# First expert's weights fetched in the last coupled step, the wait at the seam moved to GpSimd, and the weight remainders of the start spread anew

## The chip, the cores and the metric

One core of one Trainium2 chip runs the whole kernel in one launch. The metric is the device time of that launch in microseconds (us), and less is better. The kernel before was run three times: 968.25, 970.22 and 970.82 us, so its median is 970.22.

## The reference

Three layers, one after the other, all in fp32:

```python
# 1: decayed linear attention, 4 batches x 8 heads x 768 steps x 48 channels
for t in range(S):
    S_re, S_im = ar * S_re - ai * S_im + k[t] (x) v[t],  ar * S_im + ai * S_re
    y[t] = q[t] @ S_re                  # a normalised to at most 0.999 in size
# 2: dense MLP on 3072 tokens, 384 -> 2048 -> 384
h = x @ w_in;  g = max(h, 0) + alpha * min(h, 0);  x2 = g @ w_out
# 3: routed MLP: tokens with x2 @ w_skip > 0 go to one of 8 experts (384 -> 1024 -> 384)
e = argmax(x2 @ w_gate)
out = x2 + prob[e] * (relu(x2 @ w1[e]) @ w2[e])     # others: out = x2
```

## The kernel before, in words

The kernel has two blocks of instructions, one after the other; a barrier of all engines stands at the end of each. The border between them is called the seam here.

**Phase 1** (`phase1`) does the attention and the dense MLP, on 8 "halves" of 384 tokens, each of 3 chunks of 128. Step h does the attention of half h, the MLP of half h-1 and the preparation of the gates of half h+1. The order of the work of each engine is written out by hand in a function `step` of each engine. Step 0 has no MLP, steps 1 to 6 are a loop of three turns, step 7 is the last coupled step (there is no half 8 to prepare), and then the MLP of half 7 runs alone. All transfers of phase 1 are issued by SyncE, in order: q, k and v of a chunk (`load_qkv`), the decayed q and k into the layout of TensorE (`move_qk`, 10 transfers), the attention's result (`move_y`, 6), the state (`move_state`, 4), and the rows of x2, into `out` and into the scratch tensor `x2_rows` (`store_x2`, L378 and L379).

**The start of phase 1** fills the MLP's weights. Every weight is kept as two fp32r parts, a high part that ScalarE rounds and a remainder that VectorE subtracts. There are 22 pieces in a fixed order, `WEIGHT_ORDER`: in0, in1, out0, out1, in2, out2, out3, in3, out4, out5, in4, out6, out7, in5, and then out8 to out15. A piece of w_in has 512 KB and one of two staging buffers, a piece of w_out comes as two transfers of 192 KB and has one of three. So the chain of an out piece is: SyncE issues its transfers as soon as the remainder of the piece three before it is taken (`load_pack`), TensorE makes its gate columns, ScalarE makes the side-scaled copy and the high part (`split_pack`, L742 to L746), VectorE the remainder (`low_weights`, L1027). Between the pieces VectorE prepares the gates of half 0: three `scale_gates` (a reciprocal and two products, one for each chunk), seven `within`, four `across`, three `carry_products`, then `sum_products` of ScalarE's squares, `inverse` (a reciprocal, L870) and `decay_qk` (L879, L885) for the first chunk. In the kernel before VectorE takes one remainder behind each of those steps, and three, three and two behind the three `carry_products`; ScalarE makes all 22 high parts, then the three squares (L627), then `take_factors` (L623).

**The seam.** SyncE issues the last two stores of x2 and then waits for both to land; only after that does it reach the barrier that all the other engines have been waiting at.

**Phase 2** (`phase2`) routes. VectorE finds the place of each token, TensorE builds with 48 matmuls (L1274) a table of the tokens of each "slot" of 128 tokens of one expert; GpSimd gathers the rows of slot 1 by an indirect transfer into `x_in` (L1595); TensorE turns them (L1280), multiplies by w1 (L1303) and by w2 (L1317); GpSimd gathers slot s+1 while slot s is computed, and scatters finished slots (L1599). Each expert's w2 is split into high part (ScalarE, L1349) and remainder (VectorE, L1514) as well. The weights of an expert, 1.5 MB of w1 (L1248) and 1.5 MB of w2 (L1251), are issued by SyncE into one of four pairs of buffers: experts 0 to 2 at the start of phase 2, expert 3 when the table is full, because parts of the table's inputs (`in_row`, `entries`) lie in its buffers; experts 4 to 7 as experts finish. There are 13 slots in this data; the first two belong to expert 0.

```python
            for p in range(BODY - 1):
                load(0, p)
            sp.wait_ge(table_full, 1)
            load(0, BODY - 1)
```

Of the kernel before, what the change touches and what calls it, by code (L numbers as in the profile page):

```python
# [12 lines left out]
P = 128  # L13
# [99 lines left out]
def build(nc, qk, v, a, mask_in, w_in, w_pack, alpha, w_skip, w_gate, w1, w2, out, x2_rows):  # L113
    with ExitStack() as ctx:
        def sem(name):
            return ctx.enter_context(nc.semaphore(name))

        def sb(name, shape, dt=F32):
            return ctx.enter_context(nc.sbuf_tensor(name, shape, dt))

        mlp_ps = [ctx.enter_context(nc.psum_tensor(f"mlp_ps{i}", [P, 512], F32)) for i in range(2)]
        out_ps = [ctx.enter_context(nc.psum_tensor(f"out_ps{i}", [P, 512], F32)) for i in range(3)]
        att_ps = [ctx.enter_context(nc.psum_tensor(f"att_ps{i}", [P, 512], F32)) for i in range(3)]

        ident = sb("ident", [P, P])
        logits = sb("logits", [P, NT, LANES])

        phase1(nc, qk, v, a, mask_in, w_in, w_pack, alpha, w_skip, w_gate, out, x2_rows,
               mlp_ps, out_ps, att_ps, ident, logits)
        phase2(nc, w1, w2, out, x2_rows, mlp_ps, out_ps, att_ps, ident, logits)  # L130


def phase1(nc, qk, v, a, mask_in, w_in, w_pack, alpha, w_skip, w_gate, out, x2_rows,
           mlp_ps, out_ps, att_ps, ident, logits):
    with ExitStack() as ctx:
        def sem(name):
            return ctx.enter_context(nc.semaphore(name))

        def sb(name, shape, dt=F32):
            return ctx.enter_context(nc.sbuf_tensor(name, shape, dt))  # L140
# [10 lines left out]

        gates = [sb(f"gates{i}", [P, 2, NC * DM]) for i in range(2)]
        sq = sb("sq", [P, 2, NC * DM])
# [4 lines left out]

        qk_raw = sb("qk_raw", [P, 2, KT, 2, CH])
        qk_dec = sb("qk_dec", [P, 2, KT, 2, CH])  # L160
# [14 lines left out]
        g_parts = sb("g_parts", [P, 4, 2, HT], F32R)  # L175
        x2 = sb("x2", [P, NC, DL])

# [68 lines left out]
        x2_taken = sem("x2_taken")  # L246
        x2_stored = sem("x2_stored")


# [45 lines left out]
        def _(sp):  # L295
# [20 lines left out]
            def load_qkv(h, c):  # L316
# [13 lines left out]
                sp.dma_start(qk_raw[:, m, :, :, :].rearrange("p t w s -> p (t w s)"), q_src).then_inc(qk_loaded[m], 16)  # L330
                sp.dma_start(v_nat[:, m, :], v_src).then_inc(v_loaded[m], 16)
# [98 lines left out]
            with sp.Fori(0, 3) as i:  # L430
# [7 lines left out]
                step(Half(i, 2), True, True, load_but_last)  # L438
            step(Half(0, HALVES - 1), True, False, lambda: None)
            store_x2(Half(0, HALVES - 1))  # L440
            sp.wait_ge(x2_stored, val(32 * HALVES + 1))

# [151 lines left out]
        def _(act):  # L594
# [164 lines left out]
            for c in range(NC):  # L759
                pad_gates(Half(0, 0), c)  # L760
            for kind, n in WEIGHT_ORDER:
                if kind == "in":
                    split_w_in(n)
                else:
                    split_pack(n)
            for c in range(NC):
                square_products(Half(0, 0), c)
            take_factors(Half(0, 0))
            act.wait_ge(wo_lo, NF)
# [12 lines left out]
        def _(dve):  # L782
# [89 lines left out]
            def decay_qk(h, c):  # L872

                g_ = chunk_no(h, c)
                m, loads = buffer_of(h, c)
                dve.wait_ge(qk_loaded[m], loads)
                dve.wait_ge(f_inverted, val(g_ + 1))
                k_ = qk_raw[:, m, :, 1, :]
                dve.tensor_tensor(k_, k_, tiles(of_chunk(inv[:, :], c)), ALU.mult).then_inc(k_scaled, 1)  # L879
                if back(h, c):  # L880
                    dve.wait_ge(qk_moved, val(g_ * (32 * len(OP_MOVES))))
                dve.wait_ge(k_scaled, val(g_ + 1))
                for r in range(2):
                    G = tiles(of_chunk(gates[h.p][:, r, :], c)).unsqueeze(2).broadcast_to([P, KT, 2, CH])
                    last = dve.tensor_tensor(qk_dec[:, r, :, :, :], qk_raw[:, m, :, :, :], G, ALU.mult)  # L885
                last.then_inc(qk_made, 1)
# [169 lines left out]
            dve.tensor_tensor(slope_side[:, :], slope[:, :], side[:, :], ALU.mult).then_inc(alpha_made, 1)  # L1056
            scale_gates(first_h, 0)
            low_weights(0, 1)
            scale_gates(first_h, 1)
            low_weights(1, 2)  # L1060
            scale_gates(first_h, 2)
            low_weights(2, 3)
            for j in range(1, SL):
                within(first_h, j)
                low_weights(2 + j, 3 + j)
            for k in range(len(STEP_SHIFTS)):
                across(first_h, k)
                low_weights(10 + k, 11 + k)
            for part in range(3):
                carry_products(first_h, part)  # L1070
                low_weights(14 + 3 * part, 17 + 3 * part)
            for c in range(NC):
                sum_products(first_h, c)
            inverse(first_h, 0)
            decay_qk(first_h, 0)
            inverse(first_h, 1)
            inverse(first_h, 2)
# [30 lines left out]

def phase2(nc, w1, w2, out, x2_rows, mlp_ps, out_ps, att_ps, ident, logits):
    with ExitStack() as ctx:  # L1110
# [6 lines left out]

        w1_v = [sb(f"w1_sb{p}", [P, KT, FE]) for p in range(BODY)]
        w2_raw = [sb(f"w2_raw{p}", [P, NFE, DM]) for p in range(BODY)]
        w2_v = [[sb(f"w2_{part}{p}", [P, NFE, DM], F32R) for part in ("hi", "lo")] for p in range(BODY)]  # L1120
# [47 lines left out]
        scatter_at = sb("scatter_at", [P, 1], I32)  # L1168
        x_in = sb("x_in", [P, DM])
        x_kept_rows = sb("x_kept_rows", [P, 2, DM])  # L1170
        xT = sb("xT_e", [P, KT, P])
        hT = sb("hT", [P, 2, NFE, P], F32R)
        y = sb("y", [P, DM])

# [16 lines left out]
        pads_made = sem("pads_made")  # L1191
        w1_loaded = [sem(f"w1_loaded{p}") for p in range(BODY)]
        w2_loaded = [sem(f"w2_loaded{p}") for p in range(BODY)]
        w2_hi = sem("w2_hi")
# [47 lines left out]
        def _(sp):  # L1242
# [10 lines left out]

            for p in range(BODY - 1):
                load(0, p)
            sp.wait_ge(table_full, 1)
            load(0, BODY - 1)
# [318 lines left out]
        def _(pool):  # L1576
# [123 lines left out]
```

## Time and profile before

| what | value |
|---|---|
| three runs | 968.25, 970.22, 970.82 us |
| the profiled execution: its own time | 968.83 us |
| its span, first to last instruction | 966.9 us |
| what lies outside the span | 1.9 us |
| mean granted TensorE clock | 0.922 of 2.4 GHz |
| TensorE matmul, VectorE, ScalarE, GpSimd busy | 751.7, 699.2, 367.4, 51.8 us |
| phase 1, to the barrier at the seam | 0 to 766.4 us |
| routing, up to the first slot's first matmul | 766.4 to 805.1 us |
| the 13 slots | 805.1 to 966.9 us |

All times in the rows are counted from the start of the span. A line number is that of the kernel before. "SPq" is the queue of transfers that SyncE issues; the time beside such an entry is that of issuing, not that of the transfer. In the chain of waits each piece is followed back from the last instruction to what released it.

### The profile page before, as it was taken

How to read it: one execution, taken by the hardware profiler on the slowest of the kernel's cores; microseconds unless marked ns; L12 is line 12 of the kernel's file. 1: busy time of each engine (PE TensorE's matmuls, PEld its weight loads, DVE VectorE, ACT ScalarE, POOL GpSimd, SP SyncE). 2: the span in 40 equal slices, each digit the busy share in tenths (PEclk: the TensorE clock that was granted, in tenths of full speed). 3: DMA queues.
4: the chain of work that ended last, by engine and by line, in shares of the span. 5: the costliest groups of instructions: out<-in, count | busy, mean ns of one | idle time of the engine just before them, and what ended most of it. 6: DMA issues, size and time to landing. Idle time of an engine off the chain costs nothing. (4 is left out here: it accounts for less than half of the span.)

```text
span 966.9 us, 16131 instructions
## 1 busy us (share of the span) xinstructions
PE 751.7 (78%) x5478; PEld 723.3 (75%) x5479; DVE 699.2 (72%) x1231; ACT 367.4 (38%) x805; POOL 51.8 (5%) x48
## 2 busy tenths in 40 slices
PE   1343456987897989889798889979999547998786
PEld 1333456987886989788688788879999447998786
DVE  6967988988999799898899989875333373434333
ACT  5452234435434534433453353334433222322221
POOL 1000000000000000000000000000000012233122
PEclk9999567999999899999999999999999857999799
DMA  6542343243342424424242352233210393324520
GB/s 188 178 152 79 93 118 90 64 130 113 80 109 62 139 65 115 126 66 133 70 118 73 100 151 63 70 113 97 57 56 1 133 357 110 126 73 163 205 82 17
DMA packets 82433, 104.74 MB, mean 108 GB/s; under 512 B 15990, under 2 KB 68384, under 8 KB 82336
## 3 DMA queue, kind: packets, MB, share of 16 engines
q1 hardware_dynamic: 80544, 99.69, 35.2%
q0 software_dynamic: 1792, 3.76, 1.2%
q8 instruction: 61, 1.00, 0.4%
q14 instruction: 36, 0.29, 0.1%
HBM read 61.04 MB, written 12.19 MB: 76 GB/s over the span
## 5 line engine op out<-in xcount | busy, mean ns | idle before, releaser
L524 PE MATMUL out_ps<-w_out_hi,g_parts 128*128 128x394 f32 x768 | 225.3, 350 | 26.3 <-DVE g_parts L933 26.3
L514 PE MATMUL mlp_ps<-xT,w_in_hi 128*128 128x384 f32 x768 | 207.1, 351 | 20.3 <-DMA xT<-y_parts 8.6
L524 PEld LDWEIGHTS out_ps<-w_out_hi,g_parts 128*128 128x128 f32 x768 | 145.9, 193 | 30.3 <-DVE g_parts L933 30.2
L514 PEld LDWEIGHTS mlp_ps<-xT,w_in_hi 128*128 128x128 f32 x768 | 140.5, 194 | 27.5 <-issue 13.5
L928 DVE SCALAR_TENSOR_TENSOR g<-mlp_ps,slope_side,bent 128x384 f32<-128x384 f32 x128 | 78.6, 615 | 83.4 <-ACT bent L666 75.3
L524 PE MATMUL out_ps<-w_out_lo,g_parts 128*128 128x394 f32 x384 | 133.8, 348 | 0.0
L514 PE MATMUL mlp_ps<-xT,w_in_lo 128*128 128x384 f32 x384 | 131.2, 342 | 0.0
L666 ACT ACTIVATE bent<-mlp_ps,bend_size 128x384 f32<-128x384 f32 x128 | 73.7, 576 | 149.5 <-PE mlp_ps L514 149.0
L1303 PE MATMUL mlp_ps<-xT_e,w_sb 128*128 128x128 f32 x624 | 79.5, 290 | 19.3 <-issue 14.1
L1303 PEld LDWEIGHTS mlp_ps<-xT_e,w_sb 128*128 128x128 f32 x624 | 77.4, 205 | 22.1 <-issue 16.9
L672 ACT ACTIVATE g_parts<-g 128x384 fp32r<-128x384 f32 x128 | 66.2, 517 | 35.4 <-DVE g L928 35.4
L468 PE MATMUL att_ps<-ident,kq 112*128 112x112 f32 x192 | 27.5, 295 | 60.8 <-DMA kq<-qk_dec 60.8
L1544 DVE SCALAR_TENSOR_TENSOR hT<-mlp_ps,hT 128x256 fp32r<-128x256 f32 x52 | 21.8, 424 | 72.8 <-ACT hT L1375 72.8
L524 PEld LDWEIGHTS out_ps<-w_out_lo,g_parts 128*128 128x128 f32 x384 | 74.1, 193 | 0.0
L514 PEld LDWEIGHTS mlp_ps<-xT,w_in_lo 128*128 128x128 f32 x384 | 74.1, 193 | 0.0
L660 ACT ACTIVATE s_t<-s_in,f_pair 112x96 f32<-112x96 f32 x192 | 53.6, 362 | 52.9 <-DVE s_in L912 34.1
L468 PEld LDWEIGHTS att_ps<-ident,kq 112*128 112x128 f32 x192 | 22.9, 160 | 65.5 <-DMA kq<-qk_dec 55.2
L933 DVE TENSOR_TENSOR g_parts<-g,g_parts 128x384 fp32r<-128x384 f32 x128 | 70.3, 549 | 0.3
L459 PE MATMUL att_ps<-kq 112*128 112x128 f32 x384 | 60.5, 320 | 5.3 <-ACT k_back L634 5.3
L798 DVE RECIPROCAL sq<-sq 128x384 f32<-128x384 f32 x24 | 61.1, 2547 | 1.2 <-ACT sq L614 1.2
L459 PEld LDWEIGHTS att_ps<-kq 112*128 112x128 f32 x384 | 57.1, 234 | 6.4 <-ACT k_back L634 6.4
L870 DVE RECIPROCAL inv<-norms 128x384 f32<-128x384 f32 x24 | 60.0, 2529 | 0.0
(150 smaller groups left out, 1082.8 us busy)
## 6 DMA issues: line engine op xcount, KB each, us to landing
kq<-qk_dec SPq DMA_DIRECT2D x96, 144.0 KB, 3.0
w_sb<-in_w SPq DMA_DIRECT2D x8, 1536.0 KB, 7.7
w_raw<-in_w SPq DMA_DIRECT2D x8, 1536.0 KB, 12.0
gates<-in_a SPq DMA_DIRECT2D x24, 384.0 KB, 4.3
qk_raw<-in_qk SPq DMA_DIRECT2D x24, 384.0 KB, 4.2
xT<-y_parts SPq DMA_DIRECT2D x48, 144.0 KB, 2.8
v_nat<-in_v SPq DMA_DIRECT2D x24, 192.0 KB, 4.0
out<-x SPq DMA_DIRECT2D x8, 576.0 KB, 3.2
```

The lines of the kernel that those rows point to most:

```text
L459: last = pe.matmul(ps[:, n * CH:(n + 1) * CH], kq[:, slot, 1, :], kq[:, slot, 0, :], start=True, stop=True)
L468: last = pe.transpose(ps[:, n * ROWS:(n + 1) * ROWS], kq[:, PAIRS * half + n, 1, :], ident[0:ROWS, 0:ROWS])
L514: last = pe.matmul(ps[:, 0:HT], w_in_v[s][:, kk, f * P:(f + 1) * P], xT[n.p][:, kk, m, :], start=(kk == 0 and j == 0), stop=(kk == KT - 1 ...
L524: last = pe.matmul(out_ps[i][:, 0:DL], g_parts[:, f % 4, s, i * P:(i + 1) * P], w_out_v[m][:, f, :], start=(f == 0 and j == 0), stop=(f == ...
L660: last = act.activation(s_t[:, r, :, pair_, :], s_in[:, :, pair_, :], ACT.Copy, scale=f_pair[:, h.p, pair_, c, r:r + 1])
L666: act.activation(bent[:, f % 2, :], mlp_ps[f % 2][:, 0:HT], ACT.Relu, scale=bend_size[:, f:f + 1]).then_inc(bent_made, 1)
L672: act.activation(g_parts[:, f % 4, 0, :], g[:, f % 3, :], ACT.Copy).then_inc(g_hi, 1)
L798: dve.reciprocal(s1, s0).then_inc(norm_inv, 1)
L870: dve.reciprocal(of_chunk(inv[:, :], c), of_chunk(norms[:, :], c)).then_inc(f_inverted, 1)
L928: dve.scalar_tensor_tensor(out=g[:, f % 3, :], in0=mlp_ps[f % 2][:, 0:HT], scalar=slope_side[:, f:f + 1], in1=bent[:, f % 2, :], op0=ALU.m ...
L933: dve.tensor_tensor(g_parts[:, f % 4, 1, :], g[:, f % 3, :], g_parts[:, f % 4, 0, :].bitcast(F32), ALU.subtract).then_inc(g_lo, 1)
L1303: last = pe.matmul(mlp_ps[g % 2][:, (f % 2) * P:(f % 2 + 1) * P], w1_v[p][:, kk, f * P:(f + 1) * P], xT[:, kk, :], start=(kk == 0), stop=( ...
```

## The change

- The buffers of expert 0 (`arena`, two of 12 KB for each partition) are allocated outside both phases. In phase 1 they hold `gates` and `qk_raw`, both buffers of each, so that phase 2 needs no memory of its own for them; `x2` shares `rows` with `x_in`, `x_kept_rows` and `y`.
- SyncE issues the 3 MB of expert 0 in step 7, after `move_state` of chunk 1, behind a wait for the last `decay_qk`.
- SyncE no longer waits for the last stores. GpSimd waits for them in phase 2, ahead of the first gather.
- Phase 2 starts with the loads of experts 1 and 2. Expert 3 is issued when the first gather has landed instead of when the table is full.
- The clearing of `y` on GpSimd stands behind the first gather.
- In the start of phase 1 VectorE takes two remainders behind each `scale_gates` and one behind each later step; one (out14) stands between the first and the second `sum_products`, and the last (out15) behind `decay_qk` of chunk 0. ScalarE makes 20 high parts, the three squares, the last two high parts, and then `take_factors`.

```diff
+        arena = [sb(f"arena{i}", [P, KT * FE]) for i in range(2)]
+        rows = sb("rows", [P, NC * DL + DM])
+        x2_stored = sem("x2_stored")
+        first_loaded = [sem(f"first_loaded{i}") for i in range(2)]
...
-        gates = [sb(f"gates{i}", [P, 2, NC * DM]) for i in range(2)]
+        gates = [arena[i][:, 0:2 * NC * DM].rearrange("p (r x) -> p r x", r=2) for i in range(2)]
...
-        qk_raw = sb("qk_raw", [P, 2, KT, 2, CH])
+        qk_raw = [arena[i][:, 2 * NC * DM:2 * NC * DM + 2 * KT * CH].rearrange("p (t w s) -> p t w s", t=KT, w=2)
+                  for i in range(2)]
...
-        x2 = sb("x2", [P, NC, DL])
+        x2 = rows[:, 0:NC * DL].rearrange("p (i d) -> p i d", i=NC)
...
-            step(Half(0, HALVES - 1), True, False, lambda: None)
+            def fetch_first_expert():
+                sp.wait_ge(qk_made, NC * HALVES)
+                sp.dma_start(arena[0][:, :].rearrange("p (k f) -> p k f", k=KT),
+                             w1[0:1].rearrange("e (k p) f -> p (e k) f", p=P)).then_inc(first_loaded[0], 16)
+                sp.dma_start(arena[1][:, :].rearrange("p (f d) -> p f d", f=NFE),
+                             w2[0:1].rearrange("e (f p) d -> p (e f) d", p=P)).then_inc(first_loaded[1], 16)
+
+            step(Half(0, HALVES - 1), True, False, fetch_first_expert)
             store_x2(Half(0, HALVES - 1))
-            sp.wait_ge(x2_stored, val(32 * HALVES + 1))
...
-            for kind, n in WEIGHT_ORDER:
-                if kind == "in":
-                    split_w_in(n)
-                else:
-                    split_pack(n)
+            split_weights(0, 20)
             for c in range(NC):
                 square_products(Half(0, 0), c)
+            split_weights(20, 22)
             take_factors(Half(0, 0))
...
-            scale_gates(first_h, 0)
-            low_weights(0, 1)
-            scale_gates(first_h, 1)
-            low_weights(1, 2)
-            scale_gates(first_h, 2)
-            low_weights(2, 3)
+            for c in range(NC):
+                scale_gates(first_h, c)
+                low_weights(2 * c, 2 * c + 2)
             for j in range(1, SL):
                 within(first_h, j)
-                low_weights(2 + j, 3 + j)
+                low_weights(5 + j, 6 + j)
             for k in range(len(STEP_SHIFTS)):
                 across(first_h, k)
-                low_weights(10 + k, 11 + k)
+                low_weights(13 + k, 14 + k)
             for part in range(3):
                 carry_products(first_h, part)
-                low_weights(14 + 3 * part, 17 + 3 * part)
-            for c in range(NC):
-                sum_products(first_h, c)
+                low_weights(17 + part, 18 + part)
+            sum_products(first_h, 0)
+            low_weights(20, 21)
+            sum_products(first_h, 1)
+            sum_products(first_h, 2)
             inverse(first_h, 0)
             decay_qk(first_h, 0)
+            low_weights(21, 22)
...
-            for p in range(BODY - 1):
+            for p in range(1, BODY - 1):
                 load(0, p)
-            sp.wait_ge(table_full, 1)
+            sp.wait_ge(x_gathered, 16)
             load(0, BODY - 1)
...
-            pool.memset(y[:, :], 0.0).then_inc(pads_made, 1)
+            pool.wait_ge(x2_stored, 32 * HALVES + 1)
...
-            pool.wait_ge(pads_made, 2)
+            pool.wait_ge(pads_made, 1)
             pool.wait_ge(first_at, 2)
             gather()
+            pool.memset(y[:, :], 0.0).then_inc(pads_made, 1)
```

## Rows read from the trace of the kernel before

**Rows 1.** The page, transfer issues: w2's loads, count, KB each, us to landing.
```profile
w_raw<-in_w SPq DMA_DIRECT2D x8, 1536.0 KB, 12.0
```

**Rows 2.** The chain of waits from the table to slot 2: start us, us, what.
```profile
782.35 10.52 PE att_ps L1274 x48
...
794.48 8.75 DMA x_in<-x_rows,gather_at
...
805.06 7.30 PE mlp_ps L1303 x48
...
816.93 5.36 PE mlp_ps L1303 x48
```

**Rows 3.** The timeline of SyncE's queue over the seam: start us, us of issuing, line.
```profile
762.06 0.49 SPq L379 DMA_DIRECT2D x_rows<-x  x1
766.68 0.38 SPq L1248 DMA_DIRECT2D w_sb<-in_w  x1
```

**Rows 4.** SyncE's waits, 640 to 967 us: us in total, times, longest.
```profile
SPq L135 <- DMA x_rows<-x: 3.7, 1, 3.7
```

**Rows 5.** 2 us of gather 1: busy of five engines, TensorE's clock, DMA share, GB/s.
```profile
798.00:800.00 2.00, 0.00 (x0) 0.00 (x0) 0.00 (x0) 0.00 (x0) 0.00 (x0) 0.50 1.04 394
```

**Rows 6.** GpSimd's timeline: gathers 1, 2 and 8.
```profile
794.48 3.27 POOL L1595 DMA_INDIRECT x_in<-x_rows,gather_at  x1 [25.14 <-issue]
805.13 1.00 POOL L1595 DMA_INDIRECT x_in<-x_rows,gather_at  x1 [7.38 <-PE att_ps L1280]
...
868.47 1.02 POOL L1595 DMA_INDIRECT x_in<-x_rows,gather_at  x1 [4.42 <-DVE x_kept_rows L1510]
```

**Rows 7.** Issue to landing of gathers 1, 3, 5, 8 (issued 794.48, 814.62, 834.74, 868.47).
```profile
x_in<-x_rows,gather_at POOLq DMA_INDIRECT x1, 8.8
...
x_in<-x_rows,gather_at POOLq DMA_INDIRECT x1, 5.2
...
x_in<-x_rows,gather_at POOLq DMA_INDIRECT x1, 9.2
...
x_in<-x_rows,gather_at POOLq DMA_INDIRECT x1, 6.2
```

**Rows 8.** The waits of 0 to 100 us: us in total, times, longest.
```profile
PE att_ps L468 <- DMA kq<-qk_dec: 24.6, 2, 16.8
...
DVE w_out_lo L1027 <- ACT w_out_hi L746: 6.8, 6, 1.7
```

**Rows 9.** VectorE's timeline: remainders of out0 and out1, then the end of the start.
```profile
26.53 0.56 DVE L1027 TENSOR_TENSOR w_out_lo<-x,w_out_hi 128x394 fp32r<-128x394 f32 x1
...
28.42 0.57 DVE L1027 TENSOR_TENSOR w_out_lo<-x,w_out_hi 128x394 fp32r<-128x394 f32 x1
...
62.93 1.14 DVE L858 TENSOR_TENSOR gates<-norms,inv 128x945 f32<-128x945 f32 x1
...
66.72 0.57 DVE L1027 TENSOR_TENSOR w_out_lo<-x,w_out_hi 128x394 fp32r<-128x394 f32 x1 [1.00 <-ACT w_out_hi L746]
...
69.39 2.54 DVE L870 RECIPROCAL inv<-norms 128x384 f32<-128x384 f32 x1
...
72.63 1.83 DVE L885 TENSOR_TENSOR qk_dec<-qk_raw,gates 128x768 f32<-128x768 f32 x2
```

**Rows 10.** ScalarE's timeline: high part of out3, then the squares.
```profile
31.57 0.18 ACT L742 ACTIVATE x<-mlp_ps 128x10 f32<-128x10 f32 x1 [6.89 <-PE mlp_ps L569]
...
32.43 0.53 ACT L746 ACTIVATE w_out_hi<-x 128x394 fp32r<-128x394 f32 x1
...
66.59 2.29 ACT L627 ACTIVATE sq<-gates 128x768 f32<-128x768 f32 x3
```

**Rows 11.** SyncE's queue in step 7, around the place of the fetch.
```profile
683.67 2.97 SPq L367 DMA_DIRECT2D s_stack<-state  x4
695.42 4.60 SPq L359 DMA_DIRECT2D xT<-y_parts  x6
```

**Rows 12.** TensorE's timeline at the loop's way back, between experts 3 and 4.
```profile
898.45 8.35 PE L1303 MATMUL mlp_ps<-xT_e,w_sb 128*128 128x128 f32 x48 [6.80 <-issue]
```

More of the change, by code:

```diff
@@ L126, in build, with phase1 @@
         logits = sb("logits", [P, NT, LANES])
[L128 to L134, printed above, removed]
+        arena = [sb(f"arena{i}", [P, KT * FE]) for i in range(2)]
+        rows = sb("rows", [P, NC * DL + DM])
+        x2_stored = sem("x2_stored")
+        first_loaded = [sem(f"first_loaded{i}") for i in range(2)]
+        phase1(nc, qk, v, a, mask_in, w_in, w_pack, alpha, w_skip, w_gate, w1, w2, out, x2_rows,
+               mlp_ps, out_ps, att_ps, ident, logits, arena, rows, x2_stored, first_loaded)
+        phase2(nc, w1, w2, out, x2_rows, mlp_ps, out_ps, att_ps, ident, logits, arena, rows, x2_stored, first_loaded)
+def phase1(nc, qk, v, a, mask_in, w_in, w_pack, alpha, w_skip, w_gate, w1, w2, out, x2_rows,
+           mlp_ps, out_ps, att_ps, ident, logits, arena, rows, x2_stored, first_loaded):
     with ExitStack() as ctx:
@@ L246, in phase1 @@
         x2_taken = sem("x2_taken")
-        x2_stored = sem("x2_stored")
         def att(h, name, c):
@@ L329, in load_qkv @@
                     v_src = v[bass.ds(n, 1), :, :].rearrange("n p x -> (n p) x")
-                sp.dma_start(qk_raw[:, m, :, :, :].rearrange("p t w s -> p (t w s)"), q_src).then_inc(qk_loaded[m], 16)
+                sp.dma_start(qk_raw[m].rearrange("p t w s -> p (t w s)"), q_src).then_inc(qk_loaded[m], 16)
                 sp.dma_start(v_nat[:, m, :], v_src).then_inc(v_loaded[m], 16)
@@ L760, in _, with split_weights @@
                 pad_gates(Half(0, 0), c)
-            for kind, n in WEIGHT_ORDER:
-                if kind == "in":
-                    split_w_in(n)
-                else:
-                    split_pack(n)
+            def split_weights(first, last):
+                for kind, n in WEIGHT_ORDER[first:last]:
+                    if kind == "in":
+                        split_w_in(n)
+                    else:
+                        split_pack(n)
+            split_weights(0, 20)
             for c in range(NC):
                 square_products(Half(0, 0), c)
+            split_weights(20, 22)
             take_factors(Half(0, 0))
@@ L877, in decay_qk @@
                 dve.wait_ge(f_inverted, val(g_ + 1))
-                k_ = qk_raw[:, m, :, 1, :]
+                k_ = qk_raw[m][:, :, 1, :]
                 dve.tensor_tensor(k_, k_, tiles(of_chunk(inv[:, :], c)), ALU.mult).then_inc(k_scaled, 1)
@@ L884, in decay_qk @@
                     G = tiles(of_chunk(gates[h.p][:, r, :], c)).unsqueeze(2).broadcast_to([P, KT, 2, CH])
-                    last = dve.tensor_tensor(qk_dec[:, r, :, :, :], qk_raw[:, m, :, :, :], G, ALU.mult)
+                    last = dve.tensor_tensor(qk_dec[:, r, :, :, :], qk_raw[m][:, :, :, :], G, ALU.mult)
                 last.then_inc(qk_made, 1)
@@ L1106, in _, with phase2 @@
                                pattern=[[-1, P]], channel_multiplier=1).then_inc(consts, 1)
-def phase2(nc, w1, w2, out, x2_rows, mlp_ps, out_ps, att_ps, ident, logits):
+def phase2(nc, w1, w2, out, x2_rows, mlp_ps, out_ps, att_ps, ident, logits, arena, rows, x2_stored, first_loaded):
     with ExitStack() as ctx:
@@ L1115, in sb @@
             return ctx.enter_context(nc.sbuf_tensor(name, shape, dt))
-        w1_v = [sb(f"w1_sb{p}", [P, KT, FE]) for p in range(BODY)]
-        w2_raw = [sb(f"w2_raw{p}", [P, NFE, DM]) for p in range(BODY)]
+        w1_v = [arena[0][:, :].rearrange("p (k f) -> p k f", k=KT),
+                *(sb(f"w1_sb{p}", [P, KT, FE]) for p in range(1, BODY))]
+        w2_raw = [arena[1][:, :].rearrange("p (f d) -> p f d", f=NFE),
+                  *(sb(f"w2_raw{p}", [P, NFE, DM]) for p in range(1, BODY))]
         w2_v = [[sb(f"w2_{part}{p}", [P, NFE, DM], F32R) for part in ("hi", "lo")] for p in range(BODY)]
@@ L1168, in phase2 @@
         scatter_at = sb("scatter_at", [P, 1], I32)
-        x_in = sb("x_in", [P, DM])
-        x_kept_rows = sb("x_kept_rows", [P, 2, DM])
+        x_in = rows[:, NC * DL:NC * DL + DM]
+        x_kept_rows = rows[:, 0:2 * DM].rearrange("p (a d) -> p a d", a=2)
         xT = sb("xT_e", [P, KT, P])
         hT = sb("hT", [P, 2, NFE, P], F32R)
-        y = sb("y", [P, DM])
+        y = rows[:, 2 * DM:3 * DM]
         step = sem("step")
@@ L1191, in phase2 @@
         pads_made = sem("pads_made")
-        w1_loaded = [sem(f"w1_loaded{p}") for p in range(BODY)]
-        w2_loaded = [sem(f"w2_loaded{p}") for p in range(BODY)]
+        w1_loaded = [first_loaded[0], *(sem(f"w1_loaded{p}") for p in range(1, BODY))]
+        w2_loaded = [first_loaded[1], *(sem(f"w2_loaded{p}") for p in range(1, BODY))]
         w2_hi = sem("w2_hi")
```

## The prediction

> **What bounds the kernel now.** I read the chain of waits first, since it names what ends last at each point, then the timelines of the queues at the three places that the change touches, then the waits. The chain is one string over the whole span: nothing in the kernel waits for a fixed point in time, so a microsecond taken out of the string at one place is a microsecond off the end, as long as nothing that was hidden comes up beside it. Three links of the string are touched.
>
> *The start.* TensorE has nothing to do in step 0 until the decayed q and k arrive: it waits 16.8 us for them in one piece [rows 8]. Ahead of those transfers stands VectorE: last remainder at 66.72, first `inverse` at 69.39, last product of `decay_qk` done at 72.63 + 1.83 = 74.46 [rows 9]. VectorE is not busy all this time: six waits for ScalarE's high parts cost it 6.8 us [rows 8]. These waits all lie among the last eight remainders, which come in batches of three, three and two: a batch runs into the ring of three staging buffers.
>
> *The seam.* The last store of x2 is issued at 762.06 + 0.49 = 762.55; SyncE then waits 3.7 us for it to land [rows 4], and only then comes the barrier; phase 2's first load is issued at 766.68 [rows 3].
>
> *The first gather.* The table ends at 782.35 + 10.52 = 792.87. The gather is issued at 794.48 and its data is there 8.75 us later, at 803.23; the first slot's matmuls start at 805.06 [rows 2]. While it is under way, expert 3's 3 MB, issued when the table is full, fills the transfer engines (share 1.04, 394 GB/s, [rows 5]). The third gather, with no load under way, needed 5.2 us from issue to landing [rows 7]. Both had the long form of issuing, 3.27 us on GpSimd for the first, against 1.00 for the second [rows 6]; so that part stays, and the load's part is the difference.
>
> **The change part by part.**
>
> *Start of phase 1.* I work VectorE's order forward with the durations of the rows. An out remainder holds it for 0.5 us, and 1.89 together with the `within` step beside it [rows 9]. ScalarE needs 1.4 us for an out piece (31.57 to 32.96) and 2.29 for its three squares [rows 10]. The ring: out0's remainder starts at 26.53 [rows 9] and out3, next in its buffer, has its high part at 32.96 [rows 10], 6.4 us later; VectorE comes back to the buffer after at least three steps with their remainders, 5.7 us, and 7 and more where w_in pieces stand between. One remainder behind each step nearly fits that ring, three in a row do not. Before: the gates' products are done at 62.93 + 1.14 = 64.07; out14 and out15 follow, each behind a wait of about 1 us for ScalarE; the squares end at 66.59 + 2.29 = 68.88; `inverse` starts at 69.39. After: of the 6.8 us of waits, the 4.8 that stood ahead of the products go, but for one of an estimated 0.9 where the short `across` steps overtake the ring; out13's remainder now stands behind the products (0.5 less ahead). So the products are done at 64.07 - 4.8 + 0.9 - 0.5 = 59.7. Behind them ScalarE makes the squares (2.3) and out14's high part (1.4), so out14's remainder starts at 63.4: a new wait of about 2.3 us on VectorE, with `sum_products` of chunks 1 and 2 and all that follows queued behind it. Then 0.5 for the remainder and 0.5 for each of two sums: `inverse` at 65.0, `decay_qk` done at 65.0 + (74.46 - 69.39) = 70.1. Gain: 4.4 us on the path that TensorE waits for. `take_factors` comes behind out15's high part, at about 64.8, and SyncE's six transfers of factors end ahead of 70.1. ScalarE's wait for all 16 remainders ends near 70.6, and its next work, held by `inverse` before, is needed later than that. Bounds: 2.5, if the ring fails once more; 5.5, if nearly all waits went. I take 4.4.
>
> *Fetch in step 7.* SyncE finishes the state's four transfers at 683.67 + 2.97 = 686.64 and next has work at 695.42 [rows 11]. The last `decay_qk` has long been done, since `move_qk` of chunk 2 already waited for it in the same queue, so the new wait costs nothing. Two issues take 0.9 us. With 12.0 us from issue to landing for w2 [rows 1] the 3 MB are in by 699.5. Two things lie beside it: the state's transfers just ahead, needed by `values` of chunk 2 some 6 us later, and `move_y` of chunk 2 at 695.42, which may land up to 4 us later. That one is needed first by the MLP of half 7, which starts after 710. Cost 0; bound: 4 us if a transfer that TensorE waits for sticks behind it.
>
> *Seam.* The wait of 3.7 us goes, and phase 2 starts at 762.97 instead of 766.68. GpSimd's new wait for the stores is over at 766.26, more than 20 us ahead of the gather that is queued behind it. Gain 3.7; bounds 3.0 (if some engine's first instructions of phase 2 are not there yet) and 3.7.
>
> *Loads of phase 2.* Experts 1 and 2 (6 MB) start beside the tail of the stores and end some 18 us later, near 781; ScalarE's split of expert 0 no longer waits for data, that of expert 1 does, and both are done well before the first gather lands. At the first gather nothing is under way: 5.2 us in place of 8.8 [rows 7], gain 3.5. Bounds: 2.6 (8.8 less the 6.2 of gather 8, which had a load beside it) and 4.5 (no row shows less than 5.2 with the long issue, but a short one may come).
>
> *Expert 3, later.* Its 3 MB start when the first gather lands, 12 us to landing [rows 1]; its split stands in the first slot of expert 1, some 30 us later. Hidden. But gather 2 is now what meets the load. It is issued 805.13 - 803.23 = 1.9 us behind the landing of gather 1 [rows 2, 6] and wanted when TensorE has done w1 of slot 1, 805.06 + 7.30 - 803.23 = 9.1 us behind it. Gather 8, with the short issue and a load just started ahead of it, took 6.2 us [rows 6, 7]: landing 8.1 us behind, 1.0 to spare. The worst row, gather 5, took 9.2 [rows 7], which would stop TensorE for 2 us. I take 0, bound 2 lost.
>
> *Clearing of y* (0.54 us of GpSimd) moves behind the gather, where GpSimd waits anyway: 0.
>
> Sum: 4.4 + 3.7 + 3.5 = 11.6 us. From the profiled execution's 968.83 (span 966.9 and 1.9 around it) that gives 957.2. The median of the three runs, 970.22, lies 1.4 above that execution, so I forecast 958.6 for the median, 1.2% less. (A difference of about 0.3%, 2.9 us, is what a measurement of this kernel can tell from none.)
>
> **Clock.** Slot 1's w1 matmuls take 7.30 us and slot 2's 5.36 [rows 2]: the granted clock is 0.50 during the gather [rows 5], the lower level, 1.2 GHz, and rises inside slot 1. TensorE's idle stretch between table and slot 1 shrinks from 10.5 to about 7 us. I expect the same cold start. The Trainium skill (TensorE: Matmul & The Clock Gate, Part 1) says that the moment of the rise can differ from run to run of the same kernel. No run here shows that yet.
>
> **Rivals.**
>
> 1. *The gather gives nothing back (chance 0.12).* The 8.75 us could be GpSimd's long issue and the latency of the gather, and gather 2 could pay for what gather 1 gains. For: gather 1's issue of 3.27 overlaps VectorE's split, which stays. Against: gather 3 has the same long issue and lands in 5.2. Gain 4.4 + 3.7 = 8.1: 962.1. The Trainium skill (DMA: Bandwidth & Descriptors, Queues, rings and completion order) has each transfer engine take turns between the queues it has work for; by that the load would slow the gather but not hold it to its end. The trace can't tell: gather 1 landed just as the load did.
>
> 2. *The start gives nothing (0.12).* ScalarE, not VectorE, could pace the last pieces, since the two last high parts now stand behind the squares, which wait for VectorE: the new wait of 2.3 us grows to 6 and eats the gain. Against: its length is made of two measured terms. Gain 3.7 + 3.5 = 7.2: 963.0.
>
> 3. *More than the sum (0.12).* The clock rises before slot 1 and stays: 7.30 - 5.36 = 1.9 more: 956.7, or 955.6 with the upper bound of the start.
>
> 4. *Slower than before (0.04).* One mechanism: an engine runs out of instructions while a 3 MB load holds the transfer engines. The trace shows one stop of this look: TensorE stands 6.80 us with "issue" as the cause at the loop's way back [rows 12], with expert 6's load issued at that moment. The fetch now falls into step 7, where TensorE never rests, and at the seam the engines enter new code with 7 MB of stores and loads already started. A stop of 6.8 us in each of the two places costs 13.6, against 11.6 won: 972.2. It decides from 11.6 us of stops in sum. Against: over 766 to 793, with the queue as full, no engine stopped so.
>
> 5. *The change doesn't do what it says (0.02):* the wait at the seam comes back as a wait of the first gather: excluded by the 20 us above, else 962.3.
>
> **How the numbers follow.** Main case 0.58. The sum's bounds alone (start 2.5 to 5.5, seam 3.0 to 3.7, gather 2.6 to 4.5, gather 2 and step 7 up to 2 and 4 lost) give 956.5 to 968, the far end only if all fail together. The range goes to 955.0 below, where the clock gives more as well, and to 963.5 above, which holds rivals 1 and 2 and any one failed term. Faster by over 0.3% holds in the main case and rivals 1, 2, 3 and 5: 0.94. Within 0.3%: 0.03, slower 0.03, out of rival 4.
>
> **What would show it.** In the profile after: `inverse` of chunk 0 near 65.0 and TensorE's first transposes near 78 instead of 82; `out14`'s remainder behind a wait of about 2 us; x2_rows issued near 757.7; SyncE's first load of phase 2 within 0.5 us of the end of that issue; the table's end near 785; the gather landing about 5.2 us after its issue; w1 matmuls of slot 1 near 793.5; span near 955.3. Wrong would be: a wait of TensorE between 680 and 710, a wait of TensorE at the turning of slot 2's rows for gather 2, or "issue" idle in front of phase 2's first instructions.

## The result, and the profile after

The changed kernel takes 958.39 us (median of 4 runs, 955.38 to 958.93) against 969.41 before (4 runs); the ratio is 0.9891, 95% interval 0.9862 to 0.9920. The forecast was 958.6 with a range of 955.0 to 963.5. The profiled execution took 958.39 us with a span of 956.3, that is 10.4 and 10.6 less than before.

The start, VectorE's timeline (start us, us, line, what it writes and reads, the wait before it in brackets), the lines that answer to [rows 9]:

```profile
54.96 0.57 DVE L1040 TENSOR_TENSOR w_out_lo<-rows,w_out_hi 128x394 fp32r<-128x394 f32 x1 [0.66 <-ACT w_out_hi L755]
...
59.08 1.14 DVE L871 TENSOR_TENSOR arena<-norms,inv 128x945 f32<-128x945 f32 x1
...
63.88 0.57 DVE L1040 TENSOR_TENSOR w_out_lo<-rows,w_out_hi 128x394 fp32r<-128x394 f32 x1 [2.19 <-ACT w_out_hi L755]
...
65.31 2.55 DVE L883 RECIPROCAL inv<-norms 128x384 f32<-128x384 f32 x1
...
68.55 1.83 DVE L898 TENSOR_TENSOR qk_dec<-arena 128x768 f32<-128x768 f32 x2
```

The six waits of VectorE for high parts of out pieces have become two: one of 0.66 us in the ring of buffers and the new one of 2.19 for out14, ahead of the sums. A wait early in the start has grown, that for the high part of in0, from 0.28 to 1.13 us (the first line is of the kernel before):

```profile
16.15 1.23 DVE L1033 TENSOR_TENSOR w_in_lo<-gates,w_in_hi 128x1024 fp32r<-128x1024 f32 x1 [0.28 <-ACT w_in_hi L751]
16.96 2.50 DVE L1046 TENSOR_TENSOR w_in_lo<-arena,w_in_hi 128x1024 fp32r<-128x1024 f32 x2 [1.13 <-ACT w_in_hi L760]
```

`decay_qk` is done at 70.38 instead of 74.46, and TensorE's first transposes start 4.0 earlier, at 78.04:

```profile
78.04 1.75 PE L477 MATMUL att_ps<-ident,kq 112*128 112x112 f32 x8 [15.49 <-DMA kq<-qk_dec]
```

Step 7 and the seam, SyncE's queue (start us, us of issuing):

```profile
678.92 3.19 SPq L370 DMA_DIRECT2D s_stack<-state  x4
682.15 0.58 SPq L444 DMA_DIRECT2D arena<-in_w  x1
682.78 0.49 SPq L446 DMA_DIRECT2D arena<-in_w  x1
690.68 4.96 SPq L362 DMA_DIRECT2D xT<-y_parts  x6
...
757.31 0.49 SPq L382 DMA_DIRECT2D x_rows<-rows  x1
758.20 0.70 SPq L1263 DMA_DIRECT2D w_sb<-in_w  x1
...
791.37 0.37 SPq L1263 DMA_DIRECT2D w_sb<-in_w  x1
```

The fetch lies in a free stretch of the queue. From the end of issuing the last store to the first load of phase 2 it is now 0.40 us, where it was 4.13 [rows 3]: 3.73 gained. Expert 3's load starts as gather 1 lands. Gather 1 and slot 1, in the chain of waits (start us, us, what), to set beside [rows 2]:

```profile
773.87 10.52 PE att_ps L1289 x48
...
786.03 5.33 DMA rows<-x_rows,gather_at
...
793.18 7.07 PE mlp_ps L1318 x48
...
804.82 5.36 PE mlp_ps L1318 x48
...
824.96 2.01 issue
826.96 7.24 PE mlp_ps L1318 x48
```

The gather takes 5.33 us instead of 8.75, with the same long issue on GpSimd (3.25). Slot 1 starts 11.88 us earlier than before. The span is only 10.6 shorter, so the 13 slots took 1.3 us more than before: 163.1 against 161.8. The last line shows the part that grew: slot 4, the first of expert 2, takes 7.24 us for its w1 matmuls, and before it was 5.62. The first slots of experts 5, 6 and 7 do the same, 6.5 us for the four together. At the same time ScalarE waits only 7.6 us for w2 loads within the slots, where it waited 13.0. So most of it comes back, probably because the weights have more time to arrive when the slots before are longer; no run tests that. The stretches below (length; busy us and instructions of TensorE, its weight loads, VectorE, ScalarE, GpSimd; then granted clock, DMA share, GB/s) show the clock at its lower level, 1.2 GHz, there:

```profile
826.00:828.00 2.00, 1.04 (x5) 1.04 (x6) 0.19 (x1) 0.00 (x0) 0.91 (x1) 0.74 0.69 162
828.00:830.00 2.00, 2.00 (x11) 2.00 (x11) 0.00 (x0) 0.08 (x1) 0.11 (x1) 0.50 1.03 368
830.00:832.00 2.00, 2.00 (x18) 2.00 (x18) 0.45 (x2) 0.69 (x2) 0.00 (x0) 0.90 1.00 380
```

### The profile page after: what moved, and what is told of

Read it like the earlier page. It is cut to its first block and busy times, and to the rows that moved or that the text cites. A ratio compares the mean times of both kernels' runs of the same rounds, so it can differ in the third digit from the quotient of the medians.

```text
span 956.3 us, 16130 instructions
## 1 busy us (share of the span) xinstructions
PE 752.6 (79%) x5478; PEld 724.5 (76%) x5479; DVE 699.5 (73%) x1231; ACT 368.2 (39%) x805; POOL 51.8 (5%) x48
## 5 line engine op out<-in xcount | busy, mean ns | idle before, releaser
L533 PE MATMUL out_ps<-w_out_hi,g_parts 128*128 128x394 f32 x768 | 225.2, 350 | 26.2 <-DVE g_parts L946 26.2
L1318 PE MATMUL mlp_ps<-xT_e,w_sb 128*128 128x128 f32 x480 | 62.6, 295 | 8.3 <-issue 8.3
L1318 PEld LDWEIGHTS mlp_ps<-xT_e,w_sb 128*128 128x128 f32 x480 | 61.4, 211 | 10.0 <-issue 9.8
L1390 ACT ACTIVATE hT<-mlp_ps 128x256 fp32r<-128x256 f32 x52 | 20.0, 384 | 104.5 <-PE mlp_ps L1318 104.4
## 6 DMA issues: line engine op xcount, KB each, us to landing
w_raw<-in_w SPq DMA_DIRECT2D x6, 1536.0 KB, 11.6
```

The source lines that it names most:

```text
L533: last = pe.matmul(out_ps[i][:, 0:DL], g_parts[:, f % 4, s, i * P:(i + 1) * P], w_out_v[m][:, f, :], start=(f == 0 and j == 0), stop=(f == ...
L1318: last = pe.matmul(mlp_ps[g % 2][:, (f % 2) * P:(f % 2 + 1) * P], w1_v[p][:, kk, f * P:(f + 1) * P], xT[:, kk, :], start=(kk == 0), stop=( ...
```

## The experiments

All times of this section are medians of the runs of that kernel, and spans those of its one profiled execution. A table of the stages is at its end. Kernels sent together share their runs of the kernel before (967.96, 967.47, 968.46 and 967.62 us in the four groups). Only the kernels with identity matmuls (warm_table, warm_sized, warm_change, combined) add work to the changed kernel.

**undo_start**: the old order of remainders and squares in the start.

```diff
-            for c in range(NC):
-                scale_gates(first_h, c)
-                low_weights(2 * c, 2 * c + 2)
...
+            scale_gates(first_h, 0)
+            low_weights(0, 1)
...
-            split_weights(0, 20)
+            split_weights(0, 22)
             for c in range(NC):
                 square_products(Half(0, 0), c)
-            split_weights(20, 22)
```

> The changed kernel with the old order of the remainders and squares in the start. Theory (the gains add up, the start is worth about 4): the first product of decay_qk comes back to 74.5 us, TensorE's first transposes to 82, and the profiled span grows by 4 us, from 956.3 to about 960.3. Rival (the start is swallowed later): the transposes come at 82 as well, but the span stays within 1 us of 956.3.

```profile
82.61 1.76 PE L477 MATMUL att_ps<-ident,kq 112*128 112x112 f32 x8 [16.87 <-DMA kq<-qk_dec]
```

959.66 us (956.67 to 964.37, 10 runs). The transposes come back to 82.61 as both theories had it, 4.6 later than in the changed kernel. The last store ends at 761.44 instead of 757.80, 3.6 later (5.1 later than in the second profile of the changed kernel, after_again), so the start's gain lives on through phase 1. But the span was 955.3, not 960.3: the slots took 158.6 us in this execution. The rival's number came, and not by the rival's way; the span of one execution is no measure for a part of 4 us, the stages are.

**undo_seam**: SyncE's wait for the last stores put back.

```diff
             store_x2(Half(0, HALVES - 1))
+            sp.wait_ge(x2_stored, val(32 * HALVES + 1))
```

> The changed kernel with SyncE's wait for the last two stores put back at the end of phase 1. Theory: from the end of issuing the last store to the first load of phase 2 it takes 4.1 us instead of 0.4, everything behind moves by 3.7, span about 960.0. Rival (the weights of expert 0 are the point, the wait is covered): span within 1 us of 956.3.

```profile
757.99 0.49 SPq L382 DMA_DIRECT2D x_rows<-rows  x1
762.61 0.38 SPq L1264 DMA_DIRECT2D w_sb<-in_w  x1
```

4.13 us from store to load, to the hundredth the value of before; everything up to slot 1 follows by 3.7. 959.11 us (6 runs), span 957.4. The gain is shown for the stage; the span moved by 1.1 and not by 3.7, because the slots took 159.8.

**undo_e3**: expert 3 issued when the table is full.

```diff
-            sp.wait_ge(x_gathered, 16)
+            sp.wait_ge(table_full, 1)
```

> The changed kernel with expert 3 issued when the table is full, as before, so that its 3 MB run beside the first gather. Theory: the gather takes 8.8 us from issue to landing instead of 5.3, slot 1 starts 3.4 us later, span about 959.7. Rival (each transfer engine takes turns between queues, the load hardly slows the gather): 5.3 to 6.2 us, span within 1 us of 956.3. In both, gather 2 no longer meets a load and takes about 3.3 us.

```profile
784.95 8.80 DMA rows<-x_rows,gather_at
```

The gather is back at 8.80 us with nothing else changed: the load costs it 3.4 us. The rival falls. But the 3.4 us don't show in the whole: 956.86 us (4 runs), span 954.9, which is no slower than the changed kernel's 958.39 and 956.59. Slot 1 started 38.85 us behind the last store instead of 35.38, and the slots took 159.3 instead of 163.1 and 162.2. So holding expert 3 back gains its 3.4 us up to slot 1, and that it makes the launch shorter is not shown.

**undo_fetch** and **undo_fetch_again**: no fetch in step 7, expert 0 loaded first in phase 2.

```diff
-            step(Half(0, HALVES - 1), True, False, fetch_first_expert)
+            step(Half(0, HALVES - 1), True, False, lambda: None)
...
-            for p in range(1, BODY - 1):
+            for p in range(BODY - 1):
                 load(0, p)
```

> The changed kernel without the fetch in step 7: expert 0 is loaded at the start of phase 2, with experts 1 and 2; expert 3 stays behind the gather. Theory (the fetch is worth nothing by itself): 9.4 MB from 758.2 us at about 375 GB/s end near 785, just ahead of the gather's issue at 786.0, so the gather still takes 5.3 to 6 us and the span stays at 956.3 to 957. Rival (the fetch clears the way for the gather): the tail of the loads meets the gather, 1 to 3 us more, span 957.5 to 959.5.

> The kernel of undo_fetch once more, with more rounds, since its median of 954.4 us was 2 to 4 below that of the changed kernel. Theory (the fetch is worth nothing, the difference was chance in the slots' clock): the stages up to slot 1 again within 1 us of the changed kernel's, a slots' stretch that may be anything from 158.5 to 163, median 955 to 959. Rival (the fetch costs something in the slots or in step 7): median at 954.5 or less again, with a stage that is shorter by 2 us or more.

```profile
786.09 5.40 DMA rows<-x_rows,gather_at
...
793.30 7.41 PE L1318 MATMUL mlp_ps<-xT_e,arena 128*128 128x128 f32 x48 [0.81 <-ACT xT_e L1358]
```

The second line is from TensorE's timeline. The transfer engines, in the same form as the stretches above (the last two numbers are their busy share and GB/s):

```profile
785.00:786.00 1.00, 0.00 (x0) 0.00 (x0) 1.00 (x2) 0.00 (x0) 0.00 (x0) 0.50 1.01 352
786.00:787.00 1.00, 0.00 (x0) 0.00 (x0) 1.00 (x1) 0.00 (x0) 0.91 (x1) 0.50 0.11 38
```

Slot 1 starts at 793.30 (793.14 the second time) against 793.18 with the fetch: the fetch, the part that gives the change its name, gains nothing before slot 1. That is a near thing: without the fetch the loads end just as the gather is issued, at 786.09. In warm_sized and combined, further on, the gather is issued 1.8 us sooner behind the first load (26.0 us against 27.8), and there the last load would by these numbers still be under way; no run tests what the fetch is worth in those. It costs nothing in step 7 either: from the store of half 5 to that of half 6 it is 66.78 us with it and 66.71 and 66.69 without. The medians without it are 954.36 (4 runs) and 954.0 (5 runs, ratio 0.9861, interval 0.9838 to 0.9884), those with it 958.39 and 956.59. The only stage that differs is the slots' (159.5 and 158.6 against 163.1 and 162.2), and undo_start, undo_seam and undo_e3, which keep the fetch, have 158.6 to 159.8 as well. Whether the fetch costs 2 to 4 us by way of the slots, or this is chance, stays open. The intervals overlap (0.9862 to 0.9920 and 0.9861 to 0.9919 with it, 0.9821 to 0.9913 and 0.9838 to 0.9884 without), but six of the nine runs without the fetch are faster than all ten of the changed kernel, which speaks against chance alone.

**after_again**: the changed kernel once more.

> The changed kernel as it is, to see what differs between two executions of it. Theory (the stages up to slot 1 are fixed, the slots are not: the clock in the first slot after a change of expert decides): slot 1 starts within 1 us of 793.2; the stretch of the 13 slots takes 158.5 to 163 us, and the difference to the 163.1 of the profile at hand is found in first slots with 5.6 instead of 7.2 us of w1 matmuls, in part given back as waits for a w2 load. Rival (the change itself made the slots 1.3 us longer): 163 again, with the same four first slots at 7.2.

956.59 us (954.78 to 959.41, 6 runs). Slot 1 started at 791.63, the slots took 162.2, with three of the four first slots of the table below at the long form instead of four. That is nearer to the rival (the change itself lengthens the slots) than to the theory: the two profiles of the changed kernel have 163.1 and 162.2, and its forms with one part undone 158.6 to 159.8. Slot 1 itself began 1.6 earlier, more than the 1 us expected: the coupled steps of phase 1 differ between executions too, each of steps 2 to 6 between 80.3 and 83.7 us, while step 7 and the MLP of half 7 take 66.65 to 66.84 and 50.9 in every profile.

**early_split**: VectorE takes expert 0's remainder before it waits for the table.

```diff
+            split(0, 0)
             dve.wait_ge(table_full, 1)
...
-            split(0, 0)
             keep_x(1)
```

> The changed kernel with expert 0's remainder (VectorE, 3.35 us) taken before the wait for the table instead of behind the copy of the table. Theory (the issue of gather 1 takes 3.25 instead of 1.0 us because VectorE's split runs beside it, and VectorE stands idle for 4.2 us ahead of the table): gather 1 takes 1.0 us on GpSimd and 3.1 to landing, slot 1 starts 2.2 us earlier. Rival (the first gather is long because it is the first): 3.25 on GpSimd and no gain.

```profile
783.26 3.31 DMA rows<-x_rows,gather_at
...
788.38 8.57 PE mlp_ps L1318 x48
```

The split and the gather's issue in the changed kernel, then the issue here (timelines of VectorE and GpSimd):

```profile
784.87 3.35 DVE L1529 TENSOR_TENSOR w_lo<-arena,w_hi 128x3072 fp32r<-128x3072 f32 x1
786.03 3.25 POOL L1610 DMA_INDIRECT rows<-x_rows,gather_at  x1 [25.65 <-issue]
...
783.26 1.18 POOL L1610 DMA_INDIRECT rows<-x_rows,gather_at  x1 [25.63 <-issue]
```

GpSimd issues the gather in 1.18 us instead of 3.25, and it lands in 3.31: VectorE's split beside it was the cause, not that it is the first gather. In the changed kernel the issue ends 1.06 us behind the end of the split. From the table's end to slot 1 it is 6.8 us, 2.0 less. About half of it or more is handed back: the clock rises later within slot 1, whose w1 matmuls take 8.57 (8.19 in early_loads) against 7.07 and 7.58. The median is 953.18 us (951.49 to 955.32, 6 runs), 3.4 below after_again in the same group, with intervals that overlap (0.9829 to 0.9885 and 0.9861 to 0.9919). The stage accounts for 1 us or less of these 3.4; where the rest comes from is not shown.

**early_loads**: early_split, with experts 4 to 7 loaded one expert earlier.

```diff
-                    sp.wait_ge(expert_done, i * BODY + p - (BODY - 3))
+                    sp.wait_ge(expert_done, i * BODY + p - (BODY - 2))
```

> The kernel of early_split with the loads of experts 4 to 7 released one expert earlier, as soon as the expert that used the buffer is done. Theory (the slots wait for w2 of experts 4, 5 and 7 in the executions in which the first slots run at the full clock, and where they run at half clock the waits are hidden): no wait of ScalarE for a w2 load in the slots, the stretch of the slots down by 2 to 5 us from 161, median 949 to 951. Rival (the loads meet the gathers or only uncover the half-clock slots): a gather of 9 us comes late, stretch 160 to 163, median 952 to 954.

In the kernel before ScalarE waits for three w2 loads in the slots, 13.0 us, in the changed kernel 7.6 us for three; here for none. The stretch of the slots was 158.2 us, in the fastest of its six runs, but the median of 953.67 (948.65 to 957.65) is that of early_split, as the rival had it. No gain is shown; the spread is wider.

**warm_table** and **warm_sized**: identity matmuls into an unused PSUM bank fill TensorE's gaps in the routing. The numbers in the diff are those of warm_sized, which stands on top of early_split.

```diff
+            def idle_work(n):
+                for _ in range(n):
+                    pe.matmul(att_ps[2][:, 0:P], ident[:, :], ident[:, :], start=True, stop=True)
+
+            idle_work(10)
             pe.wait_ge(triangles, 2)
...
+            idle_work(36)
             for t in range(NT):
                 if t % GROUP == 0:
+                    if t:
+                        idle_work(4)
...
             last.then_inc(table_full, 1)
+            idle_work(20)
```

> The changed kernel with matmuls of the identity into an unused PSUM bank put into TensorE's gaps of the routing: 24 before the members, 64 behind their ranks, 6 ahead of the second and third group of the table, 40 behind it. Theory (the clock's lower level costs twice there): the granted clock is 1.00 through the table, the table ends 2.5 us earlier, slot 1's w1 matmuls take 5.5 instead of 7.1, in sum 3 to 4.5 us. Rival (the small matmuls of the table hold the clock down, or the added ones are in the way): clock 0.50 or a later table, gain 0 or a loss of 1 to 3.

> The kernel of early_split with a smaller filling of TensorE's gaps in the routing: each fp32 matmul of the identity is two passes of 0.11 us, so 10, 36, 4 and 20 instead of 24, 64, 6 and 40. Theory (the clock's lower level costs in table and slot 1, and the first filling was only too long): granted clock 1.00 from the ranks on, table's end 23.9 us behind the first load of phase 2 instead of 26.2, slot 1's w1 matmuls 5.6, slot 1 starts 2 us earlier, median 3 to 4 below early_split. Rival (the gaps left are too long or the filling is again in the way): 0.50 in the table, no gain.

The first filling (24, 64, 6, 40) was too long, since the trace has two passes for each of these matmuls (36 of them are the x72 below): 957.24 us (4 runs), no gain, the table ended 30.2 us behind the first load instead of 26.2. The second, on TensorE's timeline:

```profile
763.87 8.20 PE L1282 MATMUL att_ps<-ident 128*128 128x128 f32 x72
774.08 2.00 PE L1297 MATMUL att_ps<-w_raw,w_sb 128*128 128x66 f32 x16 [2.00 <-DVE w_raw L1523]
775.91 1.92 PE L1282 MATMUL att_ps<-ident 128*128 128x128 f32 x8
777.63 2.76 PE L1297 MATMUL att_ps<-w_raw,w_sb 128*128 128x66 f32 x16
780.22 1.11 PE L1282 MATMUL att_ps<-ident 128*128 128x128 f32 x8
781.17 1.90 PE L1297 MATMUL att_ps<-w_raw,w_sb 128*128 128x66 f32 x16
...
790.26 5.62 PE L1327 MATMUL mlp_ps<-xT_e,arena 128*128 128x128 f32 x48 [1.07 <-ACT xT_e L1367]
```

The last third of the table takes 1.90 us at the full clock (2.4 GHz) against 3.5, a third of 10.52, at the lower level. The filling didn't hold the clock all the way, though the expectation had 1.00 from the ranks on: in the second third (2.76 us) it was at 0.50 for a while; ahead of the first third TensorE had stood idle for 2.0 us. The table ends 23.9 us behind the first load, 2.2 earlier, and slot 1's matmuls take 5.62. So the clock's lower level in the routing is a real cost of these two stages, though GpSimd's issue came 0.5 us later and gather 2 now made TensorE wait for 0.8. For the whole it is less sure: 950.91 us (949.47 to 954.52, 5 runs), 2.3 below early_split, which ran in another group, with intervals that overlap (0.9796 to 0.9841 and 0.9829 to 0.9885).

**warm_change**: 8 such matmuls ahead of the wait at the end of each expert.

```diff
+                idle_work(8)
                 pe.wait_ge(b_done, pe.snap(until, min_val=1, max_val=NSLOT - 1))
```

> The changed kernel with 8 matmuls of the identity ahead of the wait at the end of each expert, where TensorE is idle for 2 us. Theory (that gap lets the clock fall in some executions and not in others): all first slots take 5.6 us but the one at the loop's way back, the slots' stretch is 158.5 to 160, and the spread between runs is smaller. Rival (the fall comes from something else): first slots at 7.2 as before, stretch 160 to 163.

```profile
828.26 2.05 PE L1282 MATMUL att_ps<-ident 128*128 128x128 f32 x16 [0.53 <-issue]
830.15 5.52 PE L1322 MATMUL mlp_ps<-xT_e,w_sb 128*128 128x128 f32 x48
```

Three of the four first slots took 5.52 us and the last 6.68, where the changed kernel had 7.25 four times. That the filling did this is not shown by one profile, since before, undo_start, undo_seam and undo_e3 have no long first slot without any filling. The added matmuls hold up the change itself (from slot 2's start to slot 3's it is 11.7 us, where it was 9.9): stretch 165.1, median 959.19 (954.77 to 961.14, 6 runs), 2.6 above after_again in the same group, with overlapping intervals and no smaller spread. No gain, as the rival had it.

**combined**: early_split, early_loads and warm_sized.

> early_split, early_loads and warm_sized together. Theory: the gains add, 945 to 948 us. Rival: with a shorter routing the loads of expert 3 and 4 meet and the gathers come late, 949 or more.

```profile
791.55 7.25 PE L1327 MATMUL mlp_ps<-xT_e,arena 128*128 128x128 f32 x48 [1.01 <-ACT xT_e L1367]
```

949.29 us (943.63 to 951.98, 6 runs), ratio 0.9799, interval 0.9770 to 0.9828. It has the lowest median of all and beats both kernels, but can't be told from warm_sized (950.91, same group), and it is 1.3 above the expected 945 to 948. Two things stand beside that miss: early_loads adds nothing that can be told, and slot 1's matmuls took 7.25 us in this profile, where warm_sized had 5.62 with the same filling. The clock was at 1.00 through the table, then at 0.50 again from 793 to 795 us. It leaves no work out.

The stages, in us, from the profile of each kernel (start: first transposes; store: end of issuing the last store; load: from there to the first load of phase 2; gather: issue to landing; slots: first matmul of slot 1 to the end; long: first slots with about 7.2 us of w1 matmuls, among those of experts 2, 5, 6 and 7):

| kernel | start | store | load | gather | slot 1 | slots | long |
|---|---|---|---|---|---|---|---|
| before | 82.06 | 762.55 | 4.13 | 8.75 | 805.06 | 161.8 | 0 |
| changed | 78.04 | 757.80 | 0.40 | 5.33 | 793.18 | 163.1 | 4 |
| after_again | 78.01 | 756.30 | 0.40 | 5.3 | 791.63 | 162.2 | 3 |
| undo_start | 82.61 | 761.44 | 0.40 | 5.3 | 796.73 | 158.6 | 0 |
| undo_seam | 77.96 | 758.48 | 4.13 | 5.4 | 797.61 | 159.8 | 0 |
| undo_e3 | 77.56 | 756.72 | 0.40 | 8.80 | 795.57 | 159.3 | 0 |
| undo_fetch | 77.56 | 757.87 | 0.40 | 5.40 | 793.30 | 159.5 | 1 |
| undo_fetch_again | 78.20 | 757.79 | 0.40 | 5.33 | 793.14 | 158.6 | 2 |
| early_split | 77.74 | 755.04 | 0.41 | 3.31 | 788.38 | 161.3 | 2 |

## Why the prediction was right, point by point

**The start** (4.4 forecast). 4.1 at `decay_qk`, 4.0 at the transposes. The ring's wait was 0.66 for the estimated 0.9, and the new wait behind the products 2.19 for 2.3; `inverse` started at 65.31 for 65.0. The 0.3 lies in VectorE's way to the products: they were done at 60.2, not 59.7. The sum had left out the wait for in0's high part, which grew by 0.85, and had put the ring's wait 0.24 too high. Undone, the start costs 4.6 at the transposes.

**The seam** (3.7): 3.73, and 3.73 again when the wait was put back. No engine shows a stop at its first instructions of phase 2 other than waits for another engine.

**The first gather** (3.5): 3.4, by both kernels. Rival 1, that the load does not hold up the gather, had 0.12 and falls. The Trainium skill (DMA: Bandwidth & Descriptors, Queues, rings and completion order) lets a transfer engine take turns between its queues; the runs can't show the turns themselves, only that in undo_e3 the gather landed 10.4 us behind the issue of the load ahead of it and lost 3.4 us by it. As in the kernel before, it landed just as the load did (793.75 us, the load at about 794.3).

**Gather 2 behind expert 3's load** (0, bound 2): issued at 793.25, 1.9 behind the landing of gather 1 as worked out, and TensorE waited 0.2 us for it. The step stood, with less to spare than the 1.0 forecast.

**The fetch in step 7** (0 cost): right, and its gain, which the sum never asked for, is 0 as well. The prediction left this unsaid: once expert 3 is held back, the other three experts' 9.4 MB are in by the time of the gather, with the fetch or, just barely, without. A step that costs nothing should also have been asked what it brings.

**What the sum missed.** It put nothing down for the coupled steps and the slots. The way from the transposes to the last store gave 0.7 more, and the slots took back 1.3. The measured stages, 4.02 + 0.73 + 3.73 + 3.42 - 1.28 = 10.62, make up the span's 10.6. The 0.7 is within what two executions of one kernel show (the last store at 757.80 and 756.30). For the slots that can't be said: within one kernel they differ by 0.9 (163.1 and 162.2; 159.5 and 158.6), and between the changed kernel and its forms with one part undone by 2.4 to 4.5. So it stays open whether the change itself makes the slots longer.

The three stages that the sum named gave 11.2 of the forecast 11.6. That the median came out 0.2 from the forecast is in part luck: the profiled span fell by 10.6 and the median by 11.0, and the forecast started from a median of 970.22 that four runs put at 969.41. The chances hold a slip too: the cases with a gain add up to 0.96 and not 0.94, and 0.06 was put on no gain where rival 4 has 0.04.

Rival 3 foresaw a clock that gives more; it gave less, and at a place, the change of expert, that it didn't name. "The same cold start" in slot 1 came (7.07 us), but the moment of the rise is not fixed: slot 1's matmuls took 7.07 and 7.58 us in two profiles of the same kernel. That the moment can differ from run to run is what the Trainium skill (TensorE: Matmul & The Clock Gate, Part 1) says of it, and the trace agrees.

**Rivals 2, 4 and 5** fall: the start gave its 4, no engine ran out of instructions in step 7 or at the seam, and GpSimd's new wait never held the gather. The one stop of that kind, at the loop's way back, was there before (6.80 us, [rows 12]) and is there after (7.07); in the other profiles it is 3.8 to 7.3 us.

## What to carry to other kernels

When a wait at a seam only protects a later reader, give it to that reader: here 3.7 us for one moved line. Before a large load is started, look at what small transfer on the critical chain will be behind it, and hold the load until that has landed; here that gave 3.4 us of stage, and no gain of the whole was shown for it. A microsecond won at one stage is not yet one won at the end: each of the four undone kernels shows its part at the stage (the fetch as nothing), but against 958.39 and 956.59 their medians are 959.66, 959.11, 956.86 and 954.36. For changes worth less than half a per cent measure the stage and not the span, since the rest of the kernel may differ between executions by as much.

## What the runs showed of the hardware that was not expected

- The gap of about 2 us at a change of expert sometimes lets TensorE's clock fall and sometimes does not (0 to 4 of four places in the table), at 1.6 us a time. The gap's length alone doesn't decide it: without added matmuls in the gap, in the kernels of the table, the clock fell behind gaps of 1.83 to 2.16 us and stayed up behind gaps of 1.57 to 2.24.
- The table's 48 passes keep TensorE busy for 10.5 us and yet ran at a granted clock of 0.50 throughout, before and after the change; with other matmuls in the gaps beside them it was at 1.00 all the way in warm_table and combined and for two of three parts in warm_sized, and a third of the table took 1.7 to 2.0 us instead of 3.5.
- A split on VectorE beside the gather held GpSimd's issue for 2.1 us (3.25 against 1.18), and moving it into VectorE's idle time gained 2.0 us up to slot 1, of which 1.0 to 1.5 went again as a later rise of the clock.
